# Rooms for six experts' weights, and a gating search in 16 bits, in a fused soft-MoE and top-2-MoE kernel

## The reference, cut to what matters

```
w = softmax(weight, -1)                              # 8 heads, 7 taps
x = causal 7-tap convolution of x, one set of taps per head
logits = x @ phi                                     # 32 slots, 4 for each of 8 experts
slot_input = softmax(logits, 0).T @ x
slot_out[e] = relu(slot_input[e] @ w1[e]) @ w2[e]    # F = 1024
x = softmax(logits, 1) @ slot_out
# second MoE: noisy top 2 of 8
noisy = x @ w_gate + log1p(exp(x @ w_noise)) * noise
e0, e1 = the two largest of noisy; g = softmax of these two
out = sum over k of g[k] * (relu(x @ w1[ek]) @ w2[ek])
```

## Time and profile before

| | |
|---|---|
| median of 3 runs | 976.85 us (975.1 to 979.96) |
| the profiled execution | 979.98 us, its span 978.1 us |
| TensorE busy | 905.8 us (93%) |
| VectorE busy | 625.6 us (64%) |
| ScalarE busy | 452.3 us (46%) |
| GpSimd busy | 341.7 us (35%) |
| chain that ended last | PE 87%, DVE 4%, DMA 4%, issue 2%, ACT 1% |

### The profile page before, as it was taken

The page is one execution under the profiler, slowest core; times in us unless marked ns, Lnnn a source line. Parts: engine busy times, 40 slices in busy tenths (PEclk is TensorE's granted clock), DMA queues, the critical chain, the costliest instruction groups (busy, mean ns, idle before and its releaser), DMA issues.

```text
span 978.1 us, 26085 instructions
## 1 busy us (share of the span) xinstructions
PE 905.8 (93%) x7930; PEld 726.2 (74%) x7931; DVE 625.6 (64%) x1398; ACT 452.3 (46%) x971; POOL 341.7 (35%) x362
## 2 busy tenths in 40 slices
PE   5999989996787679999999999999999999999995
PEld 5999979993463337878777777777777777777774
DVE  5132343346478968888776777677767777777773
ACT  2222221231041445555565666566656655665563
POOL 5000000001001022433455555555555656565652
PEclk9999989998656689999999999999999999999998
DMA  7447777887645212333333333333334444444441
GB/s 238 130 130 219 205 247 199 258 282 203 192 112 135 97 44 81 95 94 98 107 109 111 108 111 106 111 109 110 107 109 109 115 106 110 104 111 113 109 116 30
DMA packets 76908, 129.07 MB, mean 132 GB/s; under 512 B 10764, under 2 KB 45532, under 8 KB 74936
## 3 DMA queue, kind: packets, MB, share of 16 engines
q1 hardware_dynamic: 60696, 110.35, 38.3%
q0 software_dynamic: 15248, 17.49, 8.8%
q10 hardware_dynamic: 912, 0.52, 0.2%
HBM read 63.49 MB, written 16.86 MB: 82 GB/s over the span
## 4 chain that ended last, share of the span: by engine, by line
PE 87%; DVE 4%; DMA 4%; issue 2%; ACT 1%; POOL 0%; another core or an unknown queue 0%; ACTq 0%; SPq 0%; PEldq 0%; DVEq 0%
PE ps L1494 31%; PE ps L1498 15%; PE ps L1473 11%; PE ps L1229 10%; PE ps L1278 4%; PE ps L1280 4%; PE ps L1448 3%; PE ps L1222 3%; PE ps L1463 2%; DMA a_room<-in_moe_w 1%; PE ps L1375 1%; DMA lg<-in_moe_w 1%; PE ps L1394 1%; PE ps L1322 1%; DMA gate_room<-in_moe_w 1%
## 5 line engine op out<-in xcount | busy, mean ns | idle before, releaser
L681 ACT ACTIVATE x_ring<-ps 128x512 f16<-128x512 f32 x472 | 256.3, 598 | 215.3 <-PE ps L1473 188.2
L1494 PE MATMUL ps<-w2hl,x_ring 128*128 x1888 | 347.3, 327 | 1.1 <-DVE x_ring L1172 0.8
L1162 DVE SCALAR_TENSOR_TENSOR x_ring<-ps,x_ring 128x512 f16<-128x512 f32 x472 | 303.1, 684 | 11.5 <-ACT x_ring L681 5.1
L1494 PEld LDWEIGHTS ps<-w2hl,x_ring 128*128 128x128 f16 x1888 | 176.4, 97 | 97.8 <-issue 7.4
L553 POOL DMA_INDIRECT stage<-pay_rows,row_id x151 | 150.3, 995 | 275.9 <-PE ps L1473 159.2
L1498 PE MATMUL ps<-w2hl,x_ring 128*128 x1888 | 194.6, 246 | 1.1 <-DVE x_ring L1162 1.1
L563 POOL DMA_INDIRECT out_rows<-x_ring,row_id x151 | 169.8, 1125 | 58.4 <-issue 43.9
L1498 PEld LDWEIGHTS ps<-w2hl,x_ring 128*128 128x128 f16 x1888 | 163.1, 98 | 31.9 <-DVE x_ring L1162 1.9
L1473 PE MATMUL ps<-c,x_ring 96*128 96x128 f16 x1888 | 145.6, 220 | 0.5 <-DVE c L1155 0.5
L1155 DVE COPY c<-ps 96x256 f16<-96x256 f16 (+1 forms) x151 | 39.0, 258 | 143.7 <-PE ps L1463 124.8
L1473 PEld LDWEIGHTS ps<-c,x_ring 96*128 96x128 f16 x1888 | 122.6, 98 | 0.9 <-issue 0.9
(11 more groups left out here) (310 smaller groups left out, 658.6 us busy)
## 6 DMA issues: line engine op xcount, KB each, us to landing
x_ring<-a_room SPq DMA_DIRECT2D x236, 192.0 KB
x_ring<-in_x SPq DMA_DIRECT2D x14, 1536.0 KB, 6.9
stage<-in_moe_w SPq DMA_DIRECT2D x24, 768.0 KB, 9.6
a_room<-in_moe_w SPq DMA_DIRECT2D x12, 768.0 KB, 11.5
gate_room<-in_moe_w SPq DMA_DIRECT2D x8, 768.0 KB, 10.1
stage<-pay_rows,row_id POOLq DMA_INDIRECT x151
out_rows<-x_ring,row_id POOLq DMA_INDIRECT x151
pay_rows<-x_ring SPq DMA_DIRECT2D x1, 1904.0 KB, 6.0
```

The lines of the kernel that those rows point to most:

```text
L681: a.activation(hh[:, m % 2, 4 * half:4 * half + 4, :].rearrange("p j q -> p (j q)"), ps[:, 2 + 2 * (m % 2) + half, :], ACT.Relu).then_inc( ...
L1162: last = v.scalar_tensor_tensor(hl[:, m % 2, 4 * half:4 * half + 4, :].rearrange("p j q -> p (j q)"), ps[:, 2 + 2 * (m % 2) + half, :], 0. ...
L1494: t_.matmul(ps[:, 6 + b % 2, 0:2 * D], hh[:, m % 2, j, :], w, start=k == 0 and j == 0, stop=False)
```

## The change

The six rooms `again_rooms` replace the four through which the second MoE's `w1` went. `a3_room` is free from the end of the slot experts to the copies of the matrices. SP issues experts 0 and 1 as before, 2 to 4 at `so_ps`, 5 at `cg_ready`, and 6 and 7 (into the rooms of 0 and 1) when `a_ps` is 2.

The expert number of the search becomes a code of 16 bits, one of `CODES`, whose sums of two are all different; the class is the sum of the two codes, and `c_all` holds those sums, written by 28 memsets of GpSimd (and 8 for `e_code`) behind `consts` in place of the iotas of `e_minus` and `c_all`. The masks of `top` are 16 bits wide, in the first half of the same rooms. ScalarE copies groups 5 and 6 of the gate logits out of PSUM and takes the absolute value of part 1. `w_part(1)` stands ahead of `top(0, 1)`. The difference for the gates stands between the comparisons, and the two orders behind them.

```diff
+CODES = [s - 64.0 for s in (0, 1, 3, 7, 12, 20, 30, 44)]
+        e_code = sb("e_code", [P, E], F16)
+        pick = wins[:, 4 * T:5 * T].bitcast(F16).rearrange("p (a t) -> p a t", a=2)
+        again_rooms = [stage1[:, 0:2 * F], stage1[:, 2 * F:4 * F], stage2[:, 0:2 * F],
+                       a3_room[:, :].bitcast(F32)[:, 0:2 * F], a3_room[:, :].bitcast(F32)[:, 2 * F:4 * F],
+                       lg[:, :, :].rearrange("p t s -> p (t s)")[:, 0:2 * F]]
+        def w1_again(e):
+            return again_rooms[e % 6][0:DC, :].rearrange("p (c f) -> p c f", c=2)
...
-            for n in range(E):
-                load_w1(2 * E + n, t_w1_v)
+            for e in range(E):
+                if e == 0:
+                    sp.wait_ge(w1s_used, E + 2)
+                elif e == 2:
+                    sp.wait_ge(so_ps, E)
+                elif e == 5:
+                    sp.wait_ge(cg_ready, 1)
+                elif e == 6:
+                    sp.wait_ge(a_ps, 2)
+                sp.dma_start(w1_again(e), t_w1_v[e]).then_inc(again_in[e % 6], 16)
...
-            step(g.iota(e_minus[:, :], pattern=[[1, E]], base=-99, channel_multiplier=0,
-                        allow_small_or_imprecise_dtypes=True))
-            step(g.iota(c_all[:, :, :], pattern=[[1, NCL], [0, T]], base=-99, channel_multiplier=0,
-                        allow_small_or_imprecise_dtypes=True))
...
+            for e in range(E):
+                g.memset(e_code[:, e:e + 1], CODES[e]).then_inc(codes_ready, 1)
+            for hi in range(1, E):
+                for lo in range(hi):
+                    g.memset(c_all[:, hi * (hi - 1) // 2 + lo, :], CODES[hi] + CODES[lo]).then_inc(codes_ready, 1)
...
             for i, (lo, hi) in enumerate(GATE_PARTS):
+                if i == 1:
+                    for q in (5, 6):
+                        act.wait_ge(gl_ps, q + 1)
+                        a.activation(gl[:, 16 * q:16 * (q + 1), :].rearrange("p t e -> p (t e)"),
+                                     ps[:, 6 + q % 2, 0:32 * E], ACT.Copy).then_inc(gl_late, 1)
+                    act.wait_ge(gl_evac, 5)
+                    act.wait_ge(gl_late, 2)
+                    a.activation(ga[:, lo:hi, :], gl[:, lo:hi, E:2 * E], ACT.Abs).then_inc(z_abs, 1)
...
-                em = e_minus[:, :].unsqueeze(1).to_broadcast([P, n, E])
+                em = e_code[:, :].unsqueeze(1).to_broadcast([P, n, E])
...
-                step(v.tensor_tensor(ga[:, at, :], gc[:, at, :], mk.unsqueeze(2).to_broadcast([P, n, E]), ALU.is_equal))
-                step(v.tensor_tensor(ga[:, at, :], ga[:, at, :], em, ALU.mult))
-                step(v.tensor_reduce(pr[:, k, at], ga[:, at, :], AX.X, ALU.min))
+                step(v.tensor_tensor(ga_s, gc[:, at, :], mk.unsqueeze(2).to_broadcast([P, n, E]), ALU.is_equal))
+                step(v.tensor_tensor(ga_s, ga_s, em, ALU.mult))
+                step(v.tensor_reduce(pick[:, k, at], ga_s, AX.X, ALU.min))
                 if k == 0:
-                    step(v.tensor_tensor(gb[:, at, :], em, pr[:, 0, at].unsqueeze(2).to_broadcast([P, n, E]),
-                                         ALU.is_equal))
-                    step(v.scalar_tensor_tensor(gc[:, at, :], gb[:, at, :], -BIG, gc[:, at, :], ALU.mult, ALU.add))
+                    step(v.tensor_tensor(gb_s, em, pick[:, 0, at].unsqueeze(2).to_broadcast([P, n, E]), ALU.is_equal))
+                    step(v.scalar_tensor_tensor(gc[:, at, :], gb_s, -BIG, gc[:, at, :], ALU.mult, ALU.add))
...
-            gl_out(5)
+            dve.wait_ge(codes_ready, E + NCL)
+            dve.wait_ge(gl_ps, 6)
             top(0, 0)
-            gl_out(6)
-            dve.wait_ge(gl_evac, QGROUPS)
-            z_part(1)
+            w_part(1)
             top(0, 1)
-            w_part(1)
+            dve.wait_ge(gl_late, 2)
             noisy(1)
...
-            v.tensor_tensor(gm[:, 2, :], gm[:, 1, :], gm[:, 0, :], ALU.subtract).then_inc(m_diff, 1)
...
+            step(v.tensor_tensor(cls, pick[:, 0, :], pick[:, 1, :], ALU.add))
             for k in range(4):
...
+                if k == 1:
+                    v.tensor_tensor(gm[:, 2, :], gm[:, 1, :], gm[:, 0, :], ALU.subtract).then_inc(m_diff, 1)
+            for k in range(2):
+                step(v.tensor_tensor(pr[:, 5 + k, :], pick[:, k, :], pick[:, 1 - k, :], ALU.is_lt))
```

More of the change, by code:

```diff
@@ L117, in soft_then_top2_moe @@
         t_plus1 = sb("t_plus1", [P, T], F16)
-        e_minus = sb("e_minus", [P, E])
+        e_code = sb("e_code", [P, E], F16)
         col_iota = sb("col_iota", [P, FP + LC])
@@ L228, in cT @@
             return cT4[:, q, :] if q < 4 else (wins if q < 6 else halo)[:, q % 2 * 4 * P:(q % 2 + 1) * 4 * P]
[L230 to L231 removed]
+        w1_rooms = [stage1[:, 0:2 * F], stage1[:, 2 * F:4 * F], gate_room[:, 0:2 * F], gate_room[:, 2 * F:4 * F]]
+        again_rooms = [stage1[:, 0:2 * F], stage1[:, 2 * F:4 * F], stage2[:, 0:2 * F],
+                       a3_room[:, :].bitcast(F32)[:, 0:2 * F], a3_room[:, :].bitcast(F32)[:, 2 * F:4 * F],
+                       lg[:, :, :].rearrange("p t s -> p (t s)")[:, 0:2 * F]]
         def w1_late(n, c):
@@ L236, in w1_late @@
             return rooms[c][0:DC, :]
-        def w1_turn(n):
-            return n // WR + 1 - (1 if n >= 2 * E and n % WR < 2 else 0)
+        def w1_again(e):
+            return again_rooms[e % 6][0:DC, :].rearrange("p (c f) -> p c f", c=2)
         def w1_half(n, c, half):
@@ L249, in w1s @@
                 raise ValueError("the fifth and sixth slot experts have rooms of their own")
-            at = n % WR if n < 2 * E or n % WR < 2 else n % WR + 2
-            return w1_rooms[at][0:DC, :].rearrange("p (c f) -> p c f", c=2)
+            return w1_rooms[n % WR][0:DC, :].rearrange("p (c f) -> p c f", c=2)
         def sc(i, n=P):
@@ L263, in soft_then_top2_moe @@
         w1_late_in = [sem(f"w1_late_in{i}") for i in range(2)]
+        again_in = [sem(f"again_in{i}") for i in range(6)]
         w1s_used, w2s_used = sem("w1s_used"), sem("w2s_used")
@@ L283, in soft_then_top2_moe @@
         ctT_ps, ctT_ready, gl_ps, gl_evac = sem("ctT_ps"), sem("ctT_ready"), sem("gl_ps"), sem("gl_evac")
+        gl_late, codes_ready = sem("gl_late"), sem("codes_ready")
         z_abs, z_exp, z_w, z_ln, m_diff, m_exp = (sem(n) for n in ("z_abs", "z_exp", "z_w", "z_ln", "m_diff", "m_exp"))
@@ L370, in load_w1 @@
             def load_w1(n, src):
[L371 to L377, removed]
+                if n >= WR:
                     sp.wait_ge(w1s_used, n - WR + 1)
@@ L918, in z_part, with small @@
                 v.scalar_tensor_tensor(ga[:, at, :], z, -1.0, z, ALU.mult, ALU.max).then_inc(z_abs, 1)
+            def small(s, i):
+                lo, hi = GATE_PARTS[i]
+                return s[:, lo:hi, :].rearrange("p t e -> p (t e)").bitcast(F16)[:, 0:(hi - lo) * E].rearrange(
+                    "p (t e) -> p t e", e=E)
             def w_part(i):
@@ L966, in _ @@
             top(1, 1)
-            v.tensor_tensor(gm[:, 2, :], gm[:, 1, :], gm[:, 0, :], ALU.subtract).then_inc(m_diff, 1)
-            step(v.tensor_tensor(pr[:, 2, :], pr[:, 0, :], pr[:, 1, :], ALU.max))
-            step(v.tensor_tensor(pr[:, 3, :], pr[:, 0, :], pr[:, 1, :], ALU.min))
-            step(v.tensor_scalar(pr[:, 2, :], pr[:, 2, :], 99.0, None, ALU.add))
-            step(v.scalar_tensor_tensor(pr[:, 4, :], pr[:, 2, :], -1.0, pr[:, 2, :], ALU.add, ALU.mult))
-            step(v.scalar_tensor_tensor(cls, pr[:, 4, :], 0.5, pr[:, 3, :], ALU.mult, ALU.add))
-            for k in range(2):
-                step(v.tensor_tensor(pr[:, 5 + k, :], pr[:, k, :], pr[:, 1 - k, :], ALU.is_lt))
+            step(v.tensor_tensor(cls, pick[:, 0, :], pick[:, 1, :], ALU.add))
             part = NCL // 4
@@ L1315, in _ @@
                     else:
-                        pe.wait_ge(w1s_in[n % WR], 16 * w1_turn(n))
+                        pe.wait_ge(w1s_in[n % WR], 16 * (n // WR + 1))
                 for c in range(2):
@@ L1386, in slot_matrices @@
             def slot_matrices(i):
-                for n in (2 * E + 2 * i, 2 * E + 2 * i + 1):
-                    pe.wait_ge(w1s_in[n % WR], 16 * w1_turn(n))
+                for e in (2 * i, 2 * i + 1):
+                    pe.wait_ge(again_in[e % 6], 16 * (e // 6 + 1))
                 for c in range(2):
@@ L1394, in slot_matrices @@
                             mm = t_.matmul(ps[grp:grp + NS, i, :], slot_s[:, c, :],
-                                           w1s(2 * E + 2 * i + par)[:, c, half * BANK:(half + 1) * BANK],
+                                           w1_again(2 * i + par)[:, c, half * BANK:(half + 1) * BANK],
                                            start=c == 0, stop=c == 1, skip_group_check=True)
@@ L1402, in _ @@
             less_high(E // 2 - 1)
-            pe.wait_ge(gl_evac, QGROUPS)
+            pe.wait_ge(gl_late, 2)
             for c in range(NCL):
```

1 line of the change is left out of this document (added).

## The result

The changed kernel took 970.05 us (median of 5, 969.47 to 972.61) against 977.43 (median of 5 for the kernel before, 975.1 to 979.96). The medians differ by 7.4 us. The ratio of the two sets of executions is 0.9931, 95% interval 0.9917 to 0.9945: 5.4 to 8.1 us less. The forecast was 969.7, or 7.1 us less. The profiled execution took 969.47 us, its span 967.1.

What follows compares the result with a forecast made beforehand. With the expert loop untouched, the last two experts' weights end the gating stretch, VectorE's search nearly as late. Gains of 6.2 there and 0.9 at the start make 7.1 us: 976.85 becomes 969.7, range 966.2 to 973.8.

Steps and rivals of the forecast that it cites:

- The stage: Slot experts' gating and slot matrices, 272 to 312 us: forecast 6.2 us shorter, by shortening both weights' and VectorE's waits.
- Weights: Experts 6 and 7, issued at 287.92, land 8.8 to 9.0 us later; last pair ends at 300.0 instead of 306.45.
- VectorE: VectorE's search over gate logits: cheaper code products and moved steps start the comparisons at 300.7 instead of 304.59.
- three paths: At the stage's end, three chains of work were forecast to end together, at 304.8, 304.8 and 305.0 us.
- all 16-bit steps halved: In VectorE's search, halving them would save 1.4 us more (303.3 instead of 304.7), yet leave the forecast sum unchanged.
- The start: Before the first matmuls, removing GpSimd's c_all iota frees VectorE's last phi_r product: 0.9 us, bounds 0 to 0.95.
- the weights alone: In the gating stretch, removing only the wait for weights was said to gain under a microsecond.
- 36 memsets: GpSimd's added constants behind consts: about 0.2 us each, some 9 us from 15 to 24 us, hidden.
- Weights late: Rival: experts 6 and 7 take 12.07 us to load; gain 4.1 us with the start, 972.7 us; chance 0.12.
- VectorE stays: Rival: no 16-bit step faster, or ScalarE's copy or absolute value needs its own table; 971.8 us; chance 0.12.
- Slower: Rival: the clock stays low longer in the expert loop; 30 us longer would give 984.8 us; chance 0.05.
- the sign that it changes: Sign of a wrong prediction: the time from the totals' matmul to the end of the kernel changes.

Runs made afterwards that it cites:

- e1: The kernel before with only the six weight rooms and their waits added; 965.55 us against 968.3, ratio 0.9970.
- e2: The changed kernel with the old rooms and waits for the second MoE's w1; 968.26 us against 968.3, ratio 1.0000.
- e8: The changed kernel with separate rooms for experts 6 and 7 too, loaded in four pieces each without waiting for the slot matrices; ratio 0.9926.
- e7: The changed kernel with e_code and the masks of the search in 32 bits again; ratio 0.9929 to the kernel before.
- e4: The kernel before, unchanged, run again for a second profile; 968.88 us, ratio 1.0006.
- e9: The changed kernel with four of the eight halo transfers issued on ScalarE's queue; 961.25 us against 967.78, ratio 0.9925.
- e10: The changed kernel with eight weight rooms and the halo transfers split over two queues; 959.99 us against 967.78, ratio 0.9922.
- e6: The changed kernel with GpSimd's iota of c_all put back in its old place; 970.47 us, ratio 0.9924 to the kernel before.
- e3: The kernel before with only the iotas of e_minus and c_all moved behind GpSimd's other constants; 967.57 us against 968.3, ratio 0.9993.
- e5: The changed kernel, unchanged, run again for a second profile; 971.33 us against 978.19, ratio 0.9926.

## Why the prediction was right

**The stage, 6.2 us forecast, 6.2 to 6.6 measured** (three profiles of the changed kernel at 31.2, 31.1 and 30.9, two of before at 37.4 and 37.5). The mechanism is as it was put: two paths nearly equal before, both shortened. e1 and e2 show that neither part does it alone. e8 shows that a shorter weights' path gains at most 0.3 us, and e7 that a longer path of VectorE's costs at once.

**Weights.** TensorE went on 8.6 us after the issue at 282.72 (forecast 8.8 to 9.0). The last pair took 3.68, not 3.2. The two errors point in opposite directions, and by that luck the pair ended 12.3 after the issue where 12.1 was forecast. Counting followed 1.2 us later (1.1).

**VectorE.** From `top(0, 0)` to the class 16.75 us were forecast (283.68 to 300.43) and 278.48 to 295.23 measured, 16.75. The product, the unchanged reductions and the unchanged second equality are each as costed, and so is ScalarE's chain with its two table loads. The page named there, "VectorE: DVE Perf Modes" of the Trainium skill (sections "The perf-mode tier table (the rule you actually need)" and "Mode 2×_1P — pack two bf16 into one 32-bit read"), agrees with the 0.55 and 0.56.

**The end of the stage.** The totals' matmul was forecast 30.9 us after the first copy (305.0 less 274.09) and stood at 30.95 (299.83 less 268.88). My three paths at 304.8, 304.8 and 305.0 are really two, since TensorE's counting hangs on VectorE's first comparison. That comparison starts 26.60 us after the first copy in seven profiles (forecast 26.6), and the totals' matmul can follow at 30.6. The weights' path, which ends in the exponential, comes last in the changed kernel's first two profiles, at 30.95 and 30.85. VectorE's wait for that exponential is 0.47, 0.37 and 0.17 us in the three, and the forecast had none. For the same reason the prediction's aside that the sum would stay with all 16-bit steps halved holds only within the 0.2 us between the paths.

**The start, 0.9 us forecast.** The step held: the product fell to 528 ns in the changed kernel (the forecast said under 400). In the three profiles in which TensorE waited for `phi_r` (before, e4, e1) its second group of transposes starts at 11.56 us and its first group of taps (L1229 before, the convolution's matmuls) at 12.44 or 12.45. In the seven profiles without the iota in that place (e9 and e10 left out) it doesn't wait, and the first taps start at 11.18 to 11.92, mean 11.54, depending on when the halo landed. That is 0.9 us. The profile of e6 is left out, since the halo's landing and not the hold set its first taps.

By d_halo's exponential the difference is 1.1 us (means 141.6 and 140.5), but it holds a scatter of its own. From the first to the fourth group of taps the profiles take 6.8 to 8.2 us, with or without the iota, as the slow pace lasts shorter or longer. From the fourth group of taps to the exponential all thirteen take 121.5 to 121.6. The times of e3 (0.7, none included), of e2 and of e6 don't show the gain. That it exists at TensorE's first taps is shown; how much of it reaches the end stays open.

**Where it was wrong.** The sentence that the weights alone gain under a microsecond: 2.9 us by the time. The margin of the three paths, above. And the 36 memsets on GpSimd took 3.9 us together (14.82 to 18.72) and not some 9, which changed nothing: VectorE has nothing to do between 10.8 and 20.2 us in that profile.

**The rivals.** "Weights late" is out (8.6 us), "VectorE stays" too (0.36 and 0.42, and no load for the copy or the absolute value). "Slower" did not occur: before the loop the distance from rank to loop, first L1006 or L1023 to first L1463 or L1480, is 47.1 to 47.2 us in all profiles. In the loop the low clock lasts about as long as before: from the first transposes to the second set of eight matmuls (L1494, L1511) it is 7.0 us in before and 7.7 in the changed kernel, 6.1 to 7.2 in the five profiles without both parts and 6.6 to 7.7 in the eight with them. From the totals' matmul to the end the span has 666.9 us in before and 667.3 in the changed kernel, so the sign that it changes did not show beyond 0.4.

## What to carry to other kernels

Where two paths end within a microsecond of each other, price both ends of each, and price them where the consumer takes the first piece and not the last: that is what made "alone" 2.9 us instead of under 1. A gain then belongs to the pair of edits, and undoing either shows more than half of it lost. Look at GpSimd's long constants for what they hold on VectorE before the first matmul. And before a later time is put down to an edit, see whether the wait on which the edit acts stands in that profile at all: in e6 it didn't.

## What the runs showed of the hardware that I had not expected

- A `tensor_scalar` of 32 elements on VectorE took 2.4 to 2.7 us longer beside a GpSimd iota (2984, 2983, 2994 and 2949 ns with it, 491 to 533 without, in 13 profiles). The 28 memsets that replace its work took 3.63 us together (the iota 2.88), behind all else, at a time when VectorE had nothing to do.
- TensorE's first matmuls (some 40) run at half pace although their granted clock reads 1.00. Four transposes took 0.85 us and then 0.44. The change comes at no fixed time and no fixed distance from the first matmul: over the thirteen profiles it falls between 16.6 and 20.9 us. It makes 1.4 us of difference by the fourth group of taps.
- The second pass over x, from the first to the last start of its products (L1278 before), took 81.0 to 81.7 us in ten profiles and 82.5 to 82.7 in three (e1, e2, e5), of kernels with and without each part. All of the difference lies in its first twelve pairs of products, those of the halo. TensorE stands 3.93 us ahead of them and starts at a granted clock of 0.50 (1.2 GHz). In the ten, four to six pairs start 0.64 us or more apart before the clock reads 1.00, in the three nine pairs; after that they start 0.33 apart. From the first product with `x_ring` on, all profiles take 79.5 to 79.6 us to the first slot matmul. Why the clock rose later in the three stays open, and a difference of 1 us ahead of the pass can't be told in the total.
